# The next step's keys turned first by TensorE, and a reordered beginning, in a fused linear attention, mixture-of-experts and max-MLP kernel

## The reference

```python
# r, k, v, w: (4, 8, 768, 48); u: (8, 48)
for t in range(S):
    cur = np.einsum('bhd,bhe->bhde', u[None] * kt, vt)
    y[:, :, t] = np.einsum('bhd,bhde->bhe', rt, state + cur)
    state = wt[:, :, :, None] * state + np.einsum('bhd,bhe->bhde', kt, vt)
# x: its output as (3072, 384) tokens
xn, en = x / (norm(x) + 1e-6), expert_emb / (norm(expert_emb) + 1e-6)
idx = argmax(xn @ en.T / tau)                              # 8 experts
out[idx == e] = gate * (relu(x @ w1[e]) @ w2[e])            # 384 -> 1024 -> 384
return max(out @ m1, out @ m2, out @ m3) @ w_out            # 384 -> 768 -> 384
```

## Time and profile before

| | us |
|---|---|
| median of three runs | 729.88 (729.72 to 729.94) |
| profiled execution | 729.77 |
| its span, first to last instruction | 728.0 |
| TensorE busy | 696.6 (96%) |
| VectorE busy | 405.4 (56%) |
| ScalarE busy | 280.3 (39%) |
| GpSimd busy | 139.6 (19%) |
| attention up to the scores of step 0 | 13.4 |
| steps 0 and 1, from scores to scores | 22.5 |
| steps 2 to 13 | 114.1 |
| first product of the experts | at 187.5 |

### The profile page before, as it was taken

One profiled execution on the slowest core, in us unless ns is written; L12 is line 12 of the kernel. 1 busy time (PEld: TensorE's weight loads), 2 busy tenths in 40 slices (PEclk: granted clock), 3 DMA queues, 4 the chain that ended last, 5 costly groups with the idle time before them and its releaser, 6 DMA issues.

```text
span 728.0 us, 12780 instructions
## 1 busy us (share of the span) xinstructions
PE 696.6 (96%) x4780; PEld 622.8 (86%) x4780; DVE 405.4 (56%) x589; ACT 280.3 (39%) x593; POOL 139.6 (19%) x143
## 2 busy tenths in 40 slices
PE   7899999996999999999999999999999999999995
PEld 6788888885899999999999988988988988889875
DVE  6999999997766666555545445233233243242231
ACT  3455555574656665545345433012122021120110
POOL 6755465621522110000000000110100200101102
PEclk8999999997999999999999999999999999999999
DMA  8997777711775564343342400000000100100001
GB/s 166 212 190 165 163 154 155 197 35 39 231 229 171 169 194 131 96 125 112 103 130 89 127 0 1 12 32 1 34 11 1 44 0 1 44 0 23 23 0 44
DMA packets 148680, 66.44 MB, mean 91 GB/s; under 512 B 119560, under 2 KB 146320, under 8 KB 148624
## 3 DMA queue, kind: packets, MB, share of 16 engines
q1 hardware_dynamic: 132592, 51.43, 27.7%
q0 software_dynamic: 3072, 9.54, 4.2%
q10 hardware_dynamic: 12960, 4.73, 2.4%
HBM read 56.14 MB, written 9.54 MB: 90 GB/s over the span
## 4 chain that ended last, share of the span: by engine, by line
PE 89%; DVE 5%; issue 3%; DMA 1%; POOL 1%; ACT 0%; ACTq 0%; DVEq 0%; POOLq 0%
PE bank L1480 13%; PE bank L1481 13%; PE bank L1482 13%; PE score_banks L1480 7%; PE score_banks L1481 7%; PE score_banks L1482 7%; PE turn_banks L1481 3%; PE turn_banks L1480 3%; PE turn_banks L1482 3%; PE bank L1599 3%; PE bank L1569 3%; PE score_banks L1527 2%; PE turn_banks L1514 2%; PE bank L1585 2%; PE score_banks L1514 2%
## 5 line engine op out<-in xcount | busy, mean ns | idle before, releaser
L701 POOL DMA_INDIRECT out_dram<-o_put,slot_tok x24 | 25.2, 1050 | 438.5 <-DVE o_put L1450 438.5
L1480 PE MATMUL bank<-hh,w2h 128*128 128x432 f32 x192 | 69.3, 361 | 0.0
L1481 PE MATMUL bank<-hl,w2h 128*128 128x432 f32 x192 | 69.0, 359 | 0.0
L1482 PE MATMUL bank<-hh,w2l 128*128 128x432 f32 x192 | 69.0, 359 | 0.0
L1401 DVE SCALAR_TENSOR_TENSOR hl<-score_banks,hh 128x432 fp32r<-128x432 f32 x48 | 29.1, 607 | 66.5 <-ACT hh L915 65.5
L966 ACT CAST gh<-g 128x512 fp32r<-128x512 f32 x36 | 22.3, 620 | 105.7 <-PE bank L1482 59.7
L1480 PE MATMUL score_banks<-xh,w1h 128*128 128x432 f32 x144 | 52.9, 367 | 0.3 <-DVE xl L1363 0.3
L915 ACT ACTIVATE hh<-score_banks 128x432 fp32r<-128x432 f32 x48 | 25.5, 531 | 70.4 <-PE score_banks L1482 70.4
L1482 PE MATMUL score_banks<-xh,w1l 128*128 128x432 f32 x144 | 51.7, 359 | 0.0
L1481 PE MATMUL score_banks<-xl,w1h 128*128 128x432 f32 x144 | 51.6, 358 | 0.0
L1480 PE MATMUL bank<-moh,gh 128*128 128x384 f32 x144 | 48.5, 337 | 0.9 <-DVE gl L1468 0.9
(11 more groups left out here) (239 smaller groups left out, 1734.3 us busy)
## 6 DMA issues: line engine op xcount, KB each, us to landing
w_raw<-in_moe_w_dram SPq DMA_DIRECT2D x77, 384.0 KB, 3.3
raw_w<-in_w_dram SPq DMA_DIRECT2D x32, 144.0 KB, 3.3
raw_k<-in_k_dram SPq DMA_DIRECT2D x32, 144.0 KB, 3.4
raw_r<-in_r_dram SPq DMA_DIRECT2D x32, 144.0 KB, 3.2
vals<-in_v_dram SPq DMA_DIRECT2D x32, 144.0 KB, 2.9
x_tokens<-x_rows ACTq DMA_DIRECT2D x32, 144.0 KB, 2.8
w_raw<-in_moe_w_out_dram SPq DMA_DIRECT2D x3, 384.0 KB, 3.0
w_more<-in_moe_w_dram SPq DMA_DIRECT2D x2, 384.0 KB, 5.0
```

What stands on the lines that cost most here:

```text
L701: pool.indirect_dma_start(out=out, out_offset=bass.IndirectOffsetOnAxis(ap=slot_tok[:, n:n + 1], axis=0), in_=o_put[:, n % SB, :], in_offs ...
L1480: pe.matmul(dst, sh, mh_, start=first, stop=False)
L1481: pe.matmul(dst, sh, ml_, start=False, stop=False)
L1482: return pe.matmul(dst, sl_, mh_, start=False, stop=last)
```

## The change

It does these things:

- In each step from 1 on, TensorE turns the keys of step n+1 straight behind scores(n, 0), ahead of keys(n) and rows_of(n-1, 0), and these two change places. For step 0, keys(0) and the turning of k for step 1 stand ahead of scores(0, 0).
- Step 0 gets its own terms on the diagonals of `score` like the other steps: own_values, own_v, the products with the identity and the memset of `score` fall away. own_of(0) moves ahead of receptance_of(0), own_of(1) ahead of mask(0, 1), and mask(0, 0) waits for the diagonal.
- `u_row` has rows of 48 and no padding; its DMA is issued behind r of step 0 and moves whole rows of 384 numbers.
- The squares of the embeddings wait for the embeddings' transfer alone, and only the product with tau for tau's; two small operations become one.
- More fill products on TensorE ahead of scores(0, 1); to_rows is cleared earlier.

```diff
-    START_WARM, NEXT_WARM, LIST_WARM, TILE_WARM = 30, 10, 24, 6
+    START_WARM, LIST_WARM, TILE_WARM = 30, 24, 6
+    FILL = (10, 14, 14, 18)
...
             load(0, "r", r)
+            sp.dma_start(u_row[:, :, :].rearrange("q h d -> q (h d)"),
+                         u.rearrange("(o h) d -> o (h d)", o=1).broadcast_to([P, H * D])).then_inc(u_in, 16)
             load_w(1)
             load(1, "k", k)
             load_v(0)
-            sp.wait_ge(cleared_u, 1)
-            sp.dma_start(u_row[:, :, 0:D], u.rearrange("(o h) d -> o h d", o=1).broadcast_to([P, H, D])
-                         ).then_inc(u_in, 16)
             load(1, "r", r)
...
-            pool.memset(u_row[:, :, :], 0.0).then_inc(cleared_u, 1)
+            pool.memset(to_rows[:, :, :, :].rearrange("q x p e -> q (x p e)"), 0.0).then_inc(rows_clear, 1)
             pool.memset(vals[:, :, :, :, D:].rearrange("q n c i d -> q (n c i) d"), 0.0).then_inc(zeroed, 1)
-            pool.memset(own_v[:, :, :, D:].rearrange("q c i d -> q (c i) d"), 0.0).then_inc(zeroed, 1)
...
-            def own_values():
-
-                pool.wait_ge(own_sum, 1)
-                pool.wait_ge(v_in[0], 32)
-                pool.tensor_tensor(out=own_v[:, :, :, 0:D], in0=vals[:, 0, :, :, 0:D],
-                                   in1=own[:, 0].unsqueeze(3).broadcast_to([P, CH, 2, D]), op=ALU.mult
-                                   ).then_inc(own_ready, 1)
...
+            pool.wait_ge(pads, 3)
+            own_products(0)
             first_prefixes(0)
-            pool.memset(score[:, 0].rearrange("q c i t -> q (c i t)"), 0.0).then_inc(score_clear, 1)
-            pool.wait_ge(pads, 3)
-            pool.wait_ge(prefix_ok, 1)
-            own_products(0)
-            first_prefixes(1)
             pool.wait_ge(u_in, 16)
             own_times_u(0)
+            own_diagonal(0)
+            first_prefixes(1)
             own_products(1)
             own_times_u(1)
-            own_values()
             pool.wait_ge(prefix_ok, 2)
             own_diagonal(1)
-            for n in range(ALL - 1):
-                if n:
+            own_products(2)
+            first_prefixes(2)
+            own_times_u(2)
+            for n in range(1, ALL - 1):
+                if n > 1:
                     first_prefixes(n + 1)
...
-            act.wait_ge(small_in, 32)
+            act.wait_ge(emb_in_ok, 16)
...
-                after(dve.tensor_tensor(emb_s[:, 4:5], emb_s[:, 3:4], emb_s[:, 0:1], ALU.mult))
-                after(dve.tensor_tensor(emb_s[:, 5:6], emb_s[:, 4:5], emb_s[:, 2:3], ALU.add))
+                after(dve.scalar_tensor_tensor(out=emb_s[:, 5:6], in0=emb_s[:, 3:4], scalar=emb_s[:, 0:1],
+                                               in1=emb_s[:, 2:3], op0=ALU.mult, op1=ALU.add))
...
             def mask(n, h):
                 s = 2 * n + h
                 dve.wait_ge(scored, s + 1)
-                if n:
-                    dve.wait_ge(own_ready, n + 1)
-                else:
-                    dve.wait_ge(score_clear, 1)
+                dve.wait_ge(own_ready, n + 1)
...
             prefix_of(0)
+            own_of(0)
             receptance_of(0)
...
-                if n == 0:
-                    own_of(0)
-                elif n + 1 < ALL:
+                if n + 1 < ALL:
                     own_of(n + 1)
                 mask(n, 1)
...
-                if n == 0:
-                    own_of(1)
                 carry(n)
...
-                if n == 0:
-                    pe.wait_ge(own_ready, 1)
-                    for c in range(HALF):
-                        for i in range(2):
-                            pe.matmul(y_of(h, i, c), own_v[:, HALF * h + c, i], ident[:, :], start=False, stop=False)
...
+            def fill(times):
+                for _ in range(times):
+                    pe.matmul(bank[5][:, 0:P], ones[:, :], ones[:, :], start=True, stop=True)
+
             turn_raw(0, "w")
-            for _ in range(NEXT_WARM):
-                pe.matmul(bank[7][:, 0:P], ones[:, :], ones[:, :], start=True, stop=True)
+            fill(FILL[0])
             turn_raw(0, "k")
             turn_raw(0, "r")
             embeddings()
+            fill(FILL[1])
             turn_raw(1, "w")
+            keys(0)
+            turn_raw(1, "k")
+            fill(FILL[2])
             scores(0, 0)
+            fill(FILL[3])
             for n in range(ALL):
+                if n and n + 1 < ALL:
+                    turn_raw(n + 1, "k")
                 if n:
+                    keys(n)
                     rows_of(n - 1, 0)
-                keys(n)
-                if n + 1 < ALL:
-                    turn_raw(n + 1, "k")
                 scores(n, 1)
```

More of the change, by code:

```diff
@@ L99, in linear_attention_moe_max_mlp @@
     iota_lim = sb("iota_lim", [P, LIMS])
-    u_row = sb("u_row", [P, H, 64])
+    u_row = sb("u_row", [P, H, D])
     expert_no = sb("expert_no", [P, E])
@@ L213, in linear_attention_moe_max_mlp @@
     w_more = sb("w_more", [P, EARLY - WRAW, KD * 2 * P])
-    own_v = nc.alloc_sbuf_tensor_at("own_v", [P, CH, 2, 64], F32, offset=more_at)
-    assert 4 * CH * 2 * 64 <= cursor[0] - more_at
     assert cursor[0] <= nc.sbuf_usable_end, (cursor[0], attention_end, nc.sbuf_usable_end)
@@ L249, in sem @@
             return ctx.enter_context(nc.semaphore(name))
-        consts, cleared_u = sem("consts"), sem("cleared_u")
+        consts = sem("consts")
         pool_seq, dve_seq, act_seq = sem("pool_seq"), sem("dve_seq"), sem("act_seq")
-        small_in, u_in, warm_ok = sem("small_in"), sem("u_in"), sem("warm_ok")
+        emb_in_ok, tau_in, u_in, warm_ok = sem("emb_in_ok"), sem("tau_in"), sem("u_in"), sem("warm_ok")
         raw_in = {name: [sem(f"raw_{name}_in{i}") for i in range(RING)] for name in "wkr"}
@@ L267, in linear_attention_moe_max_mlp @@
             sem("dots_ok"), sem("dots_stored"), sem("plain_hot"), sem("plain_first"))
-        earlier_ok, fore_ok, score_clear = sem("earlier_ok"), sem("fore_ok"), sem("score_clear")
+        earlier_ok, fore_ok = sem("earlier_ok"), sem("fore_ok")
         placed, parted, apart = sem("placed"), sem("parted"), sem("apart")
@@ L591, in _ @@
                       allow_small_or_imprecise_dtypes=True).then_inc(consts, 1)
-            pool.memset(to_rows[:, :, :, :].rearrange("q x p e -> q (x p e)"), 0.0).then_inc(rows_clear, 1)
             def first_prefixes(n):
@@ L613, in own_times_u @@
                 pool.tensor_tensor(out=both, in0=both,
-                                   in1=u_row[:, 2 * p:2 * p + 2, 0:D].unsqueeze(1).broadcast_to([P, CH, 2, D]),
+                                   in1=u_row[:, 2 * p:2 * p + 2, :].unsqueeze(1).broadcast_to([P, CH, 2, D]),
                                    op=ALU.mult).then_inc(own_prod, 1)
-            def own_values():
-                pool.wait_ge(own_sum, 1)
-                pool.wait_ge(v_in[0], 32)
-                pool.tensor_tensor(out=own_v[:, :, :, 0:D], in0=vals[:, 0, :, :, 0:D],
-                                   in1=own[:, 0].unsqueeze(3).broadcast_to([P, CH, 2, D]), op=ALU.mult
-                                   ).then_inc(own_ready, 1)
             def own_diagonal(n):
@@ L663, in _ @@
                     own_times_u(n + 2)
-                if n:
-                    pool.wait_ge(prefix_ok, n + 2)
-                    own_diagonal(n + 1)
-                if n and n % PAIRS == 0:
+                pool.wait_ge(prefix_ok, n + 2)
+                own_diagonal(n + 1)
+                if n % PAIRS == 0:
                     dots_of(n // PAIRS - 1)
@@ L790, in high_chunk @@
                              raw_chunk(s, c).rearrange("q (c f) -> q c f", c=2)).then_inc(wh_ok, 1)
-            act.dma_start(emb_in[:, :], emb).then_inc(small_in, 16)
-            act.dma_start(tau_col[:, :], tau.rearrange("(a b) -> a b", a=1).broadcast_to([P, 1])).then_inc(small_in, 16)
+            act.dma_start(emb_in[:, :], emb).then_inc(emb_in_ok, 16)
+            act.dma_start(tau_col[:, :], tau.rearrange("(a b) -> a b", a=1).broadcast_to([P, 1])).then_inc(tau_in, 16)
             act.wait_ge(warm_ok, 1)
             act.activation(squares[:, 0:1], ones[0:E, 0:1], ACT.Sqrt).then_inc(act_seq, 1)
-            act.wait_ge(small_in, 32)
+            act.wait_ge(emb_in_ok, 16)
             act.wait_ge(act_seq, 1)
@@ L813, in _ @@
                     "q (x p e) -> q x p e", x=2, p=PAIRS)).then_inc(emb_ready, 1)
-            act.wait_ge(zeroed, 4)
+            act.wait_ge(zeroed, 3)
             total_of(0)
@@ L998, in embeddings @@
             def embeddings():
-                dve.wait_ge(small_in, 32)
+                dve.wait_ge(emb_in_ok, 16)
                 dve.wait_ge(emb_sq, 1)
@@ L1083, in carry @@
                 if n == 0:
-                    dve.wait_ge(zeroed, 4)
+                    dve.wait_ge(zeroed, 3)
                 if n >= 2:
@@ L1560, in mix_values @@
                 if n == 0:
-                    pe.wait_ge(zeroed, 4)
+                    pe.wait_ge(zeroed, 3)
```

2 lines of the change are left out of this document (1 added, 1 removed).

## The result

The changed kernel takes 724.6 us (median of 4 runs, 724.41 to 724.9), before 729.88: the ratio is 0.9928, interval 0.9911 to 0.9946. The profiled execution took 724.75 us with a span of 723.0 us, against 728.0 before. One run of experiment 10, 775.55 us at a granted clock of 0.841, belongs to a slower state of the chip and is left out of its ratio; all other runs are fast ones.

A forecast was written before the change was run, and what follows sets the result against it. Bound: a loop passing between TensorE and VectorE through the key turning, 9.45 us summed against 9.46 a step. Steps -5.4, beginning +0.3 and last steps 0 make -5.1 against 729.77: 724.7 us, range 722.4 to 727.8.

The forecast's parts named there:

- The loop through the key turning: Steps 2 to 13: chain from TensorE's scores through key turning to VectorE and back, 9.45 us against 9.46 measured.
- The step after: Steps 2 to 13: 8.90 us, set by TensorE's loop to the carry and back, over VectorE's own 8.79.
- The steps with expert picks: Four of the twelve steps: VectorE's two small extra operations add 0.44 us to its 8.79, making 9.23.
- The irregular idling: Steps 2 to 13: 0.59 us in all, mostly one unexplained 0.43, left as it is; 6.0 gained if it vanishes.
- The beginning: Before step 2: GpSimd's chain sets the end, suffix(2) at 25.4; 0.3 us lost, bounds 0.7 gained and 1.0 lost.
- The granted clock of steps 0 and 1: Steps 0 and 1: from 0.90 to nearer 1, counted as nothing since VectorE and GpSimd set the end.
- The diagonal: Beginning: GpSimd's diagonal operation holds up VectorE's scan, taken as 0.7 us, bounds 0 and 0.7.
- The last steps: Steps 14 and 15: counted as nothing, since keys of step 15 wait for ScalarE's copy; bounds 0 and 0.6 gained.
- The low end of the range: Whole kernel: a better beginning with step 14 keeping its gain, 722.4 us; that rival's chance 0.10.
- the first rival: Each step: GpSimd's times_u meets VectorE's prefix scan, 12 x 0.2 = 2.4 us given back, 727.1; chance 0.12.
- The spread: Each step: ScalarE's later spread holds up suffix(n+2), 12 x 0.13 = +1.6 us, total 731.7; chance 0.06.
- the 0.57 printed as "issue": VectorE's idling before keys_of: rival says its cause isn't TensorE, so no gain in the steps, 730.1 us; chance 0.08.

The follow-up runs named there:

- experiment 10: Kernel before the change with only the key turning moved up in the steps from 1 on, rows_of still ahead of keys: 723.19 us, ratio 0.9907.
- experiment 1: Kernel before the change with only TensorE's new order in steps 1 to 14 (key turning, keys, rows): 723.57 us, ratio 0.9911.
- experiment 2: Changed kernel with the old order (rows, keys, key turning) in the steps from 1 on, beginning still reworked: 730.5 us, ratio 1.0012.
- experiment 4: Changed kernel plus a VectorE memset of 192 columns ahead of the second mask in steps 2 to 14: 725.56 us, ratio 0.9943.
- experiment 5: Changed kernel plus four fill products on TensorE behind scores(n, 1) in steps 2 to 14: 725.16 us, ratio 0.9935.
- experiment 11: Changed kernel run once more, unedited (the repeat): 724.06 us, ratio 0.9923.
- experiment 9: Changed kernel without its three new groups of fill products (14, 14 and 18): 724.3 us, ratio 0.9927.
- experiment 3: Changed kernel with rows_of ahead of keys again, both behind the key turning: 723.72 us, ratio 0.9916.

## Why the prediction was right

It said 724.7 us, and 724.6 were measured, 724.06 in the repeat; of its rivals none came whole. By its steps:

- **The loop through the key turning** was the right bound. Experiments 1, 2 and 10 show that this order alone takes the steps from 114.1 to 108.0, and that nothing else in the change does.
- **The step after: right mechanism, one term mis-sized.** The prediction took 8.90, TensorE's loop to the carry and back, over VectorE's own 8.79. The steps without picks are 8.76 to 8.88 long, 8.82 on average, and experiments 4 and 5 name VectorE as the engine that sets them; the loop over TensorE is 8.71. Experiment 5, where that loop is the bound, shows its terms: key_values end at 51.47 + 0.79 - 45.44 = 6.82 of the step, 6.59 without the fill, where the prediction summed 6.78; what follows is 8.94 - 6.82 = 2.12, as summed (0.08, 0.67, 0.41, 0.09, 0.87). In step 3 of the changed kernel the first part is 51.51 + 0.79 - 45.66 = 6.64: the next start stands 0.66 behind the second rows and not 0.75, 0.75 behind r and not 0.78. So the mis-sized term is TensorE's work up to the end of key_values, by 0.14 to 0.19; no row prints why these groups stood further apart before.
- **The steps with expert picks** were put at 9.23 and are 9.27; VectorE sets these, as said. Their 0.44 of small operations were no longer covered.
- **The irregular idling** (0.59) was misread: the step with the 0.43 of the earlier trace rows, step 7, was only 0.18 longer than the usual 9.46 (83.27 to 92.91), and 0.35 stood in step 12 (130.78 to 140.59), where `keys_of` came 0.45 behind the end of the key turning and not 0.09. After the change step 12 takes 9.27 like its fellows, and step 7 takes 9.65, 0.38 more, with the same row in it:

```profile
81.59 1.77 DVE L1009 TENSOR_TENSOR_SCAN products<-decay,back_set 128x774 f32<-128x774 f32 x1 [0.43 <-issue]
```

  So about two thirds of the 0.59 stayed, but not where they had been, which the prediction had no reason for. In experiment 4 the row has no idle time (81.28) and step 7 takes 9.42 like the others with picks; why stays open. Together the steps gave 6.10 where 5.4 was expected: 8 x (8.90 - 8.82) = 0.64 from the mis-sized loop and 0.2 from this idling, less 0.15 for the steps with picks.
- **The beginning** was put at 0.3 lost, and 0.34 and 0.32 were measured in experiments 2 and 11, 0.94 in the first profile, 0.6 of it from the slow turning of w (experiment 11). The route was nearly as worked out: r*k met the scan and ended at 10.06 (9.45 expected; it started at 7.68, as r landed later than the 7.24 of before), the diagonal ran 14.12 to 15.67 (until 15.2), the scan of step 1 ended at 17.29 (16.9), own(1) waited for GpSimd at 20.50, suffix(2) came at 25.94 (25.4). The granted clock of steps 0 and 1 was to be nearer 1 and is 0.92, hardly above the 0.90 of before; as assumed, that cost nothing (experiment 9).
- **The diagonal** does hold up a scan, as assumed without a row for it: 2.46 against 1.77, 0.69 more, with 15.67 - 14.83 = 0.84 of overlap. The Trainium skill, page "SBUF — State Buffer", section "SBUF: two separate sides", has a lock for the whole instruction here; the row agrees, short of the full overlap by 0.15. This shortfall is the same for other overlaps: the prefix scan at 10.72 takes 2.68 beside times_u (10.36 to 11.77), 0.91 more for 1.05 of overlap, and the scan of the earlier trace rows 1.13 more for 1.27.
- **The last steps: counted as 0, measured +0.17,** outside the stated bounds (0 to 0.6 gained). Step 14 does get its 0.57. As the prediction worked out, keys(15) then wait for the `columns` copy, but 0.52 us where its times gave 9.97 - 9.77 = 0.20, and the stretch behind scores(15,0) grows by 0.74, for which it had no term; with rows first it doesn't grow (experiment 3). Two errors nearly cancelled.

The sum was -5.4 + 0.3 + 0; measured in the spans -6.10 + 0.94 + 0.17 = -5.0. Errors of 0.7 in the steps and 0.6 in the beginning stand against each other, so the agreement of the totals to 0.1 us is luck: in the repeat, whose beginning lost only 0.32, the same sum is -6.10 + 0.32 + 0.12 = -5.7. (The low end of the range is given as 722.4, but its own terms, 724.7 - 1.0 - 0.6 - 0.6, make 722.5.)

That GpSimd's times_u would meet the prefix scan (the first rival) did not happen: no prefix scan in the steps 2 to 14 takes more than 1.77 (three of the suffix scans take 1.83, as before). The spread did not hold up suffix either, and the 0.57 printed as "issue" was TensorE's lateness.

## What to carry over

When two engines are each busy 95% and both still idle, follow one step from start to start through both timelines and add up the spacings: where the sum hits the measured step, each group of work in that chain counts in full, and moving one of them out of it is worth more than any rework beside it. Then add up each engine's own step, since that is where the gain stops, and prove it by adding a known small piece to each engine in turn: the one on which all of it shows is the bound, and on the other the part that doesn't show is its slack. Undo the parts of a change one at a time even when it won: here two of them, keys ahead of rows and the early own sum, cost about 0.6 and 1.1 us under cover of a gain of 6. And when a run is meant to decide between two bounds, read the lengths of the steps before the total: in experiments 4 and 5 both totals fell below the range of the theory that the steps confirm, since the beginning and one irregular step had moved as well.

## What the runs showed of the hardware

- GpSimd's affine select has one input and still holds up VectorE's scan, 2.46 us instead of 1.77. A memset on GpSimd, which only writes, doesn't: in the kernel before it ran from 9.61 to 10.99, and the scan that started at 10.46 took 1.77. The other way round a scan already running holds up GpSimd: its product took 2.38 and not 1.41.
- VectorE's memset of 192 columns is shown with 0.22 us but lengthens the step by 0.15 only; four small bf16 products are shown with 0.40 us on TensorE and move the next group by 0.23. A piece of work costs its spacing, not its length.
- The turning of the first w took 0.84 us in one execution of the changed kernel and 1.51 in another, and between these two the whole beginning moved by 0.6 us. The records show the granted clock at 1.00 in both. Six such turnings take 1.54 us where it is recorded as 0.50 (experiment 9, at 19.11), so a low clock that the records miss would fit, but no run shows it.
